# The narrow pair of token tiles is processed first instead of last in a fused attention and two-FFN kernel

## What is computed

```python
qn = q / (norm of q over the tokens + 1e-6)      # per channel
kn = k / (norm of k over the tokens + 1e-6)
a  = softmax(kn.T @ qn / tau)                    # 256 x 256
x  = v @ a                                       # 6016 x 256
h  = x @ w_in1;  x = (h - tanh(h)) @ w_out1      # part 1
h  = x @ w_in2;  out = where(h > 0, h, exp(min(h, 0)) - 1) @ w_out2   # part 2
```

## Time and profile before

| what | value |
|---|---|
| median of three runs | 1035.09 us (1032.75 to 1037.13) |
| profiled execution, its own time | 1032.56 us |
| span, first to last instruction of it | 1030.8 us |
| TensorE busy | 99% of the span, 4574 matmuls |
| VectorE busy | 820.0 us, 80% |
| ScalarE busy | 765.1 us, 74% |
| DMA, mean | 45 GB/s |

### The profile page before, as it was taken

The page is one execution under the profiler, slowest core; times in us unless marked ns, Lnnn a source line. Parts: engine busy times, 40 slices in busy tenths (PEclk is TensorE's granted clock), DMA queues, the critical chain, the costliest instruction groups (busy, mean ns, idle before and its releaser), DMA issues.

```text
span 1030.8 us, 13739 instructions
## 1 busy us (share of the span) xinstructions
PE 1025.0 (99%) x4574; PEld 858.0 (83%) x4574; DVE 820.0 (80%) x1362; ACT 765.1 (74%) x1360; POOL 0.8 (0%) x7
## 2 busy tenths in 40 slices
PE   9999999999999999999999999999999999999998
PEld 8868888888888888888998888888888888888997
DVE  5899977777867776777998888887887887787776
ACT  6687776666766666767878878777878787778775
POOL 0000000000000000000000000000000000000000
PEclk9999999999999999999999999999999999999999
DMA  9932012003003001012222002102101201200202
GB/s 356 295 74 41 1 41 42 1 22 62 1 10 69 0 1 42 1 41 72 62 57 92 1 1 62 21 1 60 22 1 42 42 1 37 42 1 1 41 0 37
DMA packets 117830, 46.24 MB, mean 45 GB/s; under 512 B 100352, under 2 KB 108544, under 8 KB 117760
## 3 DMA queue, kind: packets, MB, share of 16 engines
q1 hardware_dynamic: 113616, 43.99, 16.2%
q10 hardware_dynamic: 4144, 1.38, 0.5%
HBM read 33.03 MB, written 12.32 MB: 44 GB/s over the span
## 4 chain that ended last, share of the span: by engine, by line
PE 98%; DVE 1%; issue 0%; ACT 0%; POOL 0%; ACTq 0%; POOLq 0%
PE r_ps L325 17%; PE r_ps L327 16%; PE r_ps L326 16%; PE x_ps L325 6%; PE x_ps L326 6%; PE x_ps L327 6%; PE z_ps L325 4%; PE z_ps L327 4%; PE z_ps L326 4%; PE y_ps L326 2%; PE q_ps L325 2%; PE y_ps L327 2%; PE y_ps L325 2%; PE q_ps L327 2%; PE q_ps L326 2%; PE x_ps L332 2%
## 5 line engine op out<-in xcount | busy, mean ns | idle before, releaser
L594 ACT ACTIVATE g_hi<-g 128x512 fp32r<-128x512 f32 (+1 forms) x384 | 236.5, 616 | 143.0 <-DVE g L839 58.4
L692 DVE TENSOR_TENSOR g_lo<-g,g_hi 128x512 fp32r<-128x512 f32 (+1 forms) x384 | 259.5, 676 | 49.5 <-ACT g_hi L594 40.9
L325 PE MATMUL r_ps<-g_hi,w_out_hi 128*128 128x512 f32 (+1 forms) x768 | 296.0, 385 | 0.0
L327 PE MATMUL r_ps<-g_hi,w_out_lo 128*128 128x512 f32 (+1 forms) x768 | 295.7, 385 | 0.0
L326 PE MATMUL r_ps<-g_lo,w_out_hi 128*128 128x512 f32 (+1 forms) x768 | 295.7, 385 | 0.0
L325 PEld LDWEIGHTS r_ps<-g_hi,w_out_hi 128*128 128x128 f32 x768 | 144.2, 188 | 27.5 <-issue 0.4
L327 PEld LDWEIGHTS r_ps<-g_hi,w_out_lo 128*128 128x128 f32 x768 | 144.2, 188 | 27.1
L326 PEld LDWEIGHTS r_ps<-g_lo,w_out_hi 128*128 128x128 f32 x768 | 144.2, 188 | 26.7
L325 PE MATMUL x_ps<-t_hi,w_ops 128*128 128x512 f32 (+1 forms) x288 | 111.3, 387 | 0.1
L326 PE MATMUL x_ps<-t_lo,w_ops 128*128 128x512 f32 (+1 forms) x288 | 111.0, 385 | 0.0
L327 PE MATMUL x_ps<-t_hi,w_ops 128*128 128x512 f32 (+1 forms) x288 | 110.9, 385 | 0.0
(11 more groups left out here) (109 smaller groups left out, 1484.3 us busy)
## 6 DMA issues: line engine op xcount, KB each, us to landing
v_blocks<-v_dram SPq DMA_DIRECT2D x40, 128.0 KB, 3.1
x_scratch<-side SPq DMA_DIRECT2D x20, 256.0 KB, 2.0
vt<-x_scratch SPq DMA_DIRECT2D x20, 256.0 KB, 3.6
out_dram<-v_blocks SPq DMA_DIRECT2D x80, 64.0 KB, 1.9
k_ring<-k_dram SPq DMA_DIRECT2D x9, 512.0 KB, 10.0
q_ring<-q_dram SPq DMA_DIRECT2D x9, 512.0 KB, 10.8
w_out_raw<-moe_w_out_dram SPq DMA_DIRECT2D x1, 2048.0 KB, 15.6
w_raw<-moe_w_in_dram SPq DMA_DIRECT2D x16, 128.0 KB, 2.5
```

The source lines that it names most:

```text
L325: nc.tensor.matmul(ps, w_hi, m_hi, start=start, stop=False, skip_group_check=True)
L327: return nc.tensor.matmul(ps, w_lo, m_hi, start=False, stop=stop, skip_group_check=True)
L594: nc.scalar.activation(g_hi[b][n % DEPTH[b]][:, 0:width], g[b][:, 0:width], ACT.Copy).then_inc(g_rounded[b], 1)
L692: return nc.vector.tensor_tensor(lo, x, hi.bitcast(F32), ALU.subtract)
```

## The change

One line. The list of widths has its narrow pair at the front. Everything else follows from the list: pair 0 (quads 0 to 7, and 48 to 55 in part 2, where it is pair 6) has 448 columns per tile, and pair 5 (quads 40 to 47, and 88 to 95) has 512. The tokens of each pair move with it.

```diff
 TILE = 512
-WIDTH = [512] * 5 + [448]
+WIDTH = [448] + [512] * 5
 PAIRS = len(WIDTH)
 TOKEN0 = [2 * sum(WIDTH[:p]) for p in range(PAIRS)]
```

## The result

Over twelve runs each, the changed kernel takes 1035.56 us in the median (1034.57 to 1037.90) and the kernel before 1032.86 (1032.14 to 1037.13). The ratio is 1.0025, with a 95% interval of 1.0015 to 1.0034: some 2.6 us slower. That is clear of zero and within the 0.5% that were called no change. The kernel before came out 2.2 us lower over twelve runs than over the three first shown, so the predicted 1036.2 lies near the measured 1035.56 partly by that; the difference is the better measure, +1.25 us predicted and +2.6 measured. The profiled execution of the changed kernel took 1035.17 us with a span of 1033.34, 2.58 us over the span before (1030.76).

A forecast was written before the change was run, and what follows sets the result against it. TensorE, busy 99% of the span, was taken as the bound; -0.2 + 0.3 + 0.1 + 0.6 + 0.45 = +1.25 us on the median 1035.09 gave 1036.3, centred at 1036.2, range 1033.0 to 1039.8.

The forecast's parts named there:

- The matmuls: zero: All quads: 80 of 512 and 16 of 448 columns before and after, so 17.3 us only move between pairs.
- third sign: TensorE's matmul step: the prediction is wrong if it differs from 0.203 and 0.227 us.
- Pair 0, quads 2 to 7: Six narrow quads with weight work in part 1: +0.1 us of waits, bounds 0 and 2.4.
- Rival 1: Pairs 0 and 6: VectorE becomes the metronome, 0.4 us for 15 of 16 quads, +6.25 us in all; chance 0.05.
- Quads 0 and 1: Start of part 1, where TensorE already waits: +0.3 us of new waiting, bounds 0 and +0.8.
- Pair 6: Quads 48 to 51, start of part 2: lost cover gives +0.6 us, bounds -0.42 and +2.0.
- rival 2: Start of part 2: its waits vanish, -0.42 in place of +0.6, +0.2 us in all; chance 0.25.
- Prologue and end: Before quad 0, an earlier second scaling of the scores, -0.2 us; at the end, longer last operations and stores, +0.45 us.
- Moved transfers: Loads and stores of other sizes in the same number and order: nothing, as TensorE's matmuls cover them.

The follow-up runs named there:

- a_late: Changed kernel with the w_out split of quads 2 to 7 moved later in VectorE's queue, behind h22 and blocks 22 and 12; 1.0015 times the kernel before.
- b_dve: Kernel before with one more VectorE operation of 320 columns (some 0.40 us) in each of quads 2 to 6; 1.0013 times the kernel before.
- b_act: Kernel before with one more ScalarE operation of 384 columns (some 0.40 us) in each of quads 2 to 6; 1.0015 times the kernel before.
- b_both: Kernel before with both a VectorE operation of 320 columns and a ScalarE operation of 384 added in each of quads 2 to 6; 1.0041 times the kernel before.
- half_first: Changed kernel with widths 480, 480, then four of 512, in place of 448 and five of 512; 1.0023 times the kernel before.
- narrow1: Changed kernel with the narrow pair in second place: widths 512, 448, then four of 512; 1.0013 times the kernel before.
- after_again: The changed kernel run once more with no edit; one run, 1034.82 us.
- a_pool: Changed kernel with the six splits of w_out of quads 2 to 7 computed by GpSimd instead of VectorE; 1.0036 times the kernel before.

## Why the prediction was right, and where not

**Sign and size.** No change within 0.5%, slightly slower: both held, and 1035.56 lies in the range. That the number came so near is luck. The difference was forecast at half its size, and two of its terms missed in opposite directions: quads 2 to 7 by +2.0 us, pair 6 by -0.8. The median before then fell by 2.2 us with more runs. (The ends of the range, too, do not follow from their own recipe: 1035.09 + 3.5 and 1.5 to 2 more is 1040.1 to 1040.6, not 1039.8.)

**The matmuls: zero.** Nearly. 80 and 16 quads of the two widths, 10.20 and 9.12, as said. But 9.12 was taken for a constant of the width, on two narrow pairs that both had it. The step of 448 columns has a second value, 0.2066, and pair 0 ran in it for 155 matmuls: 0.6 us that no term held. By the prediction's own third sign, a step other than 0.203 and 0.227, it was wrong there.

**Pair 0, quads 2 to 7: the step that failed.** Predicted 0.1 us with a bound of 2.4, found 1.5 of waits. The cover lost was right (0.4 us per quad), and the 2.07 us in all lie within the bound. The value was chosen by the nearest row, quad 45, a narrow quad with weight work and no wait. That row was the wrong neighbour: quad 45 has its weight splits beside one operation on the next pair's tiles, where quads 5 and 6 have three. Quads 2 and 6, which the text itself had put at 9.08 and 9.16 of 9.12, were the right ones. And the reserve of 1.00 before P6 in quad 6 was read as if only that quad drew on it; in the changed kernel it is 0.74, 0.32, 0.65 and 0.46 us in quads 2 to 5 and gone in quad 6. Even so, busy time gives the places only roughly. Quads 3 and 5 of the kernel before:

```profile
87.97:98.17 10.20, 10.20 (x46) 8.45 (x45) 9.61 (x15) 7.94 (x16) 0.00 (x0) 1.00 0.38 60
...
108.37:118.57 10.20, 10.20 (x46) 8.45 (x45) 9.48 (x15) 7.66 (x15) 0.00 (x0) 1.00 0.00 1
```

Quad 3 had VectorE busy for longer than quad 5, and yet TensorE came to wait in quad 5 and not in quad 3: the order in the queues counts beside the sum, as a_late shows. b_dve, b_act and b_both show that 0.4 us in a queue makes such waits at full width, and half_first that 0.1 does not.

**Rival 1** had the right place and a price too high: VectorE is the metronome in three quads of 15, not in all. By its own sign, quads 2 to 7 at 9.3 or more, it holds in five of six, but in 3 and 4 the time is the slow step and not a wait for VectorE. The sentence of the Trainium skill beside it (VectorE: DVE Perf Modes, the section on the TRN2 errata) was borne out in direction: an operation gave back 0.068 us of 0.687, a tenth, for an eighth of the columns. But the fixed part is the smaller half of the matter: ten operations without one would give back at most 10 x 0.687 / 8 = 0.86 us against TensorE's 1.08. So of the 0.40 us lost per quad the fixed part explains at most 0.18, and the rest is there because the weight work and the next pair's tiles, some 3 of VectorE's 9.8 us in the fullest quads, do not have the pair's width. Its `6 + FD` for a matmul does not fit: by it an estimate is (6 + 448) / 2.4 GHz = 189 ns, and the rows have 203 and 207.

**Quads 0 and 1.** +0.3 predicted, +0.38 found; the first second product of quad 1 starts 0.41 us late instead of 0.16.

**Pair 6.** +0.6 predicted, -0.2 found, though 0.2 us of waits is left in quads 50 and 51. The term went half the way of rival 2: with pair 5 at full width, quad 48 starts with 1.26 us of reserve before P6 instead of 1.12, and in quad 49 there are still 0.76 left where there were 0.28. The bound of -0.42 was right, the value not. narrow1, with pair 5 and pair 6 both wide, has no wait in quad 49 and the same 0.3 us in quad 50, so the wide pair 5 is what helps, by 0.17 us there. It does not make that wait go away.

**Prologue and end.** -0.2 predicted; from the first scaling of the scores (44.85 before, 45.25 after) to quad 0 the time fell from 13.77 to 13.28 us. The mechanism that was named is there: the second scaling comes 3.19 us behind the first where it was 3.43, 0.24 us of the 0.27 counted. The other 0.25 us are not assigned, and the start of quad 0 varies by more than the term from execution to execution (-0.09 between these two profiles), so the size stays open. The end: +0.45 predicted, 0.37 found against the one profile before, and less than 0.1 against two others with a narrow last pair.

**Moved transfers.** Nothing waited for a load in either part.

## What to carry to other kernels

Narrower tiles take less off the side engines than off TensorE, in part since each operation has a fixed part and in part since some of their work does not have the tile's width; so the narrow tile belongs where the side queues are emptiest, and the last place has a shorter end besides (by 0.06 to 0.4 us here). To price lost cover, take the reserve in front of each wait, quad by quad, and the fullest neighbour, not the mean busy share: 0.1 us per quad cost nothing, 0.4 us on one engine 0.75 to 1.07 us, and 0.4 us on both 2.76.

## What the runs showed of the hardware beside this

- The step of back-to-back matmuls of 448 columns, each with its own weight load, has two values, 0.2027 and 0.2066 us, at a granted clock of 1.00. The fast one held for up to 315 steps (quads 41 to 47 of the kernel before), the slow one for up to 133 (changed kernel, 84 to 112 us). It changed at waits in the changed kernel (at 84, 112, 117 and 122 us), and without a wait in quads 3 and 54 of after_again and in quad 61 of narrow1. What selects it is open; it was worth 0.6 us in one execution of the changed kernel and 0.7 in the other. 480 columns ran at 0.2167 and 512 at 0.2267, so 0.2066 is the value in line with these two and 0.2027 the odd, better one.
- A two-input subtraction on GpSimd of 128 x 512 takes 1.33 us in the mean of six, and a VectorE split beside it goes from 0.62 to 1.42 us (a_pool).
